# Where TensorE issues the fresh-state products of an attention chunk: behind the other products, or ahead of them

## Time and profile before

| | us |
|---|---|
| median of three runs | 808.82 |
| the three runs | 806.82, 808.82, 809.68 |
| the profiled execution, its own time | 804.45 |
| its span, first to last instruction | 802.5 |
| PE busy in it | 776.2 |
| DVE busy | 536.0 |
| ACT busy | 344.2 |
| POOL busy | 180.3 |

### The profile page before, as it was taken

One profiled execution on the slowest core, in us unless ns is written; L12 is line 12 of the kernel. 1 busy time (PEld: TensorE's weight loads), 2 busy tenths in 40 slices (PEclk: granted clock), 3 DMA queues, 4 the chain that ended last, 5 costly groups with the idle time before them and its releaser, 6 DMA issues.

```text
span 802.5 us, 12138 instructions
## 1 busy us (share of the span) xinstructions
PE 776.2 (97%) x4624; PEld 731.4 (91%) x4624; DVE 536.0 (67%) x1026; ACT 344.2 (43%) x676; POOL 180.3 (22%) x202
## 2 busy tenths in 40 slices
PE   3999999999999999999999999999999999999996
PEld 2769998899999999999999999999999999999996
DVE  7788989865768657666666676676675765553432
ACT  3567554343344343353443443345334444334332
POOL 5515313222213302122212122122221221100000
PEclk9999999999999999999999999999999999999998
DMA  8960222032021221030220311203202030000000
GB/s 227 304 216 1 60 60 60 1 89 60 1 60 30 60 59 31 30 90 1 60 52 9 90 23 37 60 1 89 60 1 60 14 77 30 1 1 29 2 1 33
DMA packets 18849, 43.52 MB, mean 54 GB/s; under 512 B 2272, under 2 KB 14688, under 8 KB 18400
## 3 DMA queue, kind: packets, MB, share of 16 engines
q1 hardware_dynamic: 15136, 34.81, 17.5%
q10 hardware_dynamic: 3648, 7.87, 2.8%
HBM read 37.95 MB, written 4.72 MB: 53 GB/s over the span
## 4 chain that ended last, share of the span: by engine, by line
PE 78%; DVE 2%; ACT 0%; issue 0%; DVEq 0%; ACTq 0%
PE BANKS L1133 55%; PE MISC L1133 20%; PE BANKS L1310 2%; PE MISC L1157 1%; PE MISC L1150 1%; DVE RL L965 0%; DVE Rraw L958 0%; DVE att L818 0%; DVE W2L L976 0%; DVE ki L826 0%; DVE A L839 0%; ACT RH L691 0%; ACT Rraw L687 0%; DVE X2L L982 0%; DVE RL L967 0%
## 5 line engine op out<-in xcount | busy, mean ns | idle before, releaser
L687 ACT ACTIVATE Rraw<-BANKS 128x384 f32<-128x384 f32 x128 | 62.9, 491 | 217.8 <-PE BANKS L1133 217.6
L958 DVE TENSOR_TENSOR Rraw<-BANKS,Rraw 128x384 f32<-128x384 f32 x128 | 71.0, 555 | 118.9 <-ACT Rraw L687 118.8
L1133 PE MATMUL BANKS<-RH,W4H 128*128 128x384 f32 x384 | 135.7, 353 | 0.9 <-DVE RL L965 0.8
L1133 PE MATMUL BANKS<-X2H,W3H 128*128 128x384 f32 x384 | 130.7, 340 | 0.2 <-DVE X2L L982 0.2
L1133 PE MATMUL BANKS<-X2L,W3H 128*128 128x384 f32 x384 | 129.4, 337 | 0.0
L1133 PE MATMUL BANKS<-X2H,W3L 128*128 128x384 f32 x384 | 129.3, 337 | 0.0
L1133 PE MATMUL BANKS<-RH,W4L 128*128 128x384 f32 x384 | 129.2, 337 | 0.0
L1133 PE MATMUL BANKS<-RL,W4H 128*128 128x384 f32 x384 | 129.1, 336 | 0.0
L691 ACT ACTIVATE RH<-Rraw 128x384 fp32r<-128x384 f32 x128 | 67.2, 525 | 94.0 <-DVE Rraw L958 94.0
L965 DVE TENSOR_TENSOR RL<-Rraw,RH 128x384 fp32r<-128x384 f32 x128 | 79.2, 619 | 22.5 <-ACT RH L691 22.5
L826 DVE RECIPROCAL ki<-att 112x128 f32<-112x128 f32 x96 | 89.1, 936 | 0.0
(11 more groups left out here) (137 smaller groups left out, 1486.2 us busy)
## 6 DMA issues: line engine op xcount, KB each, us to landing
att<-rkw SPq DMA_DIRECT2D x48, 288.0 KB, 4.8
out<-OUT SPq DMA_DIRECT2D x8, 576.0 KB, 6.2
rtok<-r_tok SPq DMA_DIRECT2D x22, 192.0 KB, 4.7
ktok<-k_tok SPq DMA_DIRECT2D x22, 192.0 KB, 4.8
vtok<-v_tok SPq DMA_DIRECT2D x22, 192.0 KB, 5.0
W3raw<-w_in ACTq DMA_DIRECT2D x1, 3072.0 KB, 14.6
W4raw<-w_out ACTq DMA_DIRECT2D x1, 3072.0 KB, 18.5
W1raw<-w_in SPq DMA_DIRECT2D x1, 1536.0 KB, 11.5
```

Of the source, the lines that this page charges most:

```text
L687: nc.scalar.activation(Rraw[:, fp % 2, :], PR[fp % 2][:, 0:ST], ACT.Copy, scale=0.01).then_inc(act_slope, 1)
L958: nc.vector.tensor_tensor(Rraw[:, fp % 2, :], PR[fp % 2][:, 0:ST], Rraw[:, fp % 2, :], ALU.max).then_inc(dve_relu, 1)
L1133: return nc.tensor.matmul(dst, lhsT, rhs, start=start, stop=stop, skip_group_check=True)
```

## The change

For the chunks that `item` serves, PE's slot 5 first waits for the tokens and, where the chunk has a fresh state, for the masks of all four pairs; it issues the fresh-state products there, and `attend` behind them. The waits inside `attend` stay, though those for tokens and masks are then already met. Chunks 0 to 2 and the last of each batch keep their order.

```diff
                 if s == 5:
                     wait(pe, act_keT, chunks(b, m, 1, 1))
+                    wait_tok(pe, b, m)
+                    if m % CPB < CPB - 1:
+                        wait(pe, dve_masked, chunks(b, m, PAIRS, PAIRS))
+                        fresh_state(b, m)
                     attend(b, m)
-                    if m % CPB < CPB - 1:
-                        fresh_state(b, m)
```

## The result

The changed kernel takes 814.7 us (median of nine runs, 811.3 to 815.74) against 808.82 for the kernel before on the same chip (nine runs, 804.62 to 810.12). The ratio is 1.0076, 95% interval 1.006 to 1.0091: 6.1 us slower, 4.9 to 7.4. Sign, place and range held; some 1.7 us were not in the sum, and 6.1 lies above the sum's own upper bound of 4.9.

A forecast was written before the change was run, and what follows sets the result against it. TensorE, busy 776.2 of 802.5 us, was taken to bound the kernel. Stalls of 2.45 + 0.97 + 0.55 + 0.41 = 4.4 us on 808.82 gave 813.2, range 809.8 to 815.4.

The forecast's parts named there:

- order of the products, 17 blocks: Same products and weights in another order in slot 5: zero cost, bounded at 0.3 us either way.
- nine blocks with 0.35 or more in hand: Chunks 7, 8, 10, 13, 14, 16, 19, 20, 22: masks end early enough before the first load, so zero cost.
- chunks 9, 12, 15, 18, 21: First chunk of each superstep: first load moves from 0.37 before the masks' end to 0.12 behind, 0.49 each, 2.45 us.
- chunk 4: Masks end 0.92 us after the first load; with 0.12 release 1.04, less 0.07 for the second load: 0.97.
- chunk 6, the wait: TensorE, already idle 1.66 us, waits for the second mask too: first load 0.60 later, taken as 0.55 us.
- chunk 3, the late sum: VectorE gets Y later, so the state starts 0.45 later and TensorE's first expert load moves 0.41 us.
- The release takes 0.12, not 0.05: Time from a mask's end to the load it releases: 0.12 us from chunk 6, 0.05 from chunk 1 as low bound.
- Chunk 6 gives little back at 160.39: TensorE's 0.28 us wait for VectorE's RL could take back up to 0.28 of chunk 6's delay; most comes back.
- A load given back for each wait: Loads pulled ahead past a waiting load would return 0.11 us at each of seven waits, sum 3.6; not adopted.
- Rival 1, taken back: Later TensorE waits (XL, 160.39, behind chunk 9 and its like) absorb 3.2 us, leaving 1.2: 810.0; chance 0.13.
- Rival 2, not felt: Loads run far ahead or release is free; only chunks 3, 4, 6 show parts, under 1.5 us: 810; chance 0.05.
- Rival 3, VectorE's lead: Chunk 4's stall lets VectorE get ahead for good, later waits vanish: -0.7 us, 808.1; chance 0.04.

The follow-up runs named there:

- e3_in_hand: Kernel before with the changed order only in the nine chunks whose masks are 0.35 us or more in hand; 809.31 us against 808.86, ratio 1.0011.
- e2: Changed kernel with the added waits kept at the head of slot 5, but the fresh-state products back behind the A products; 815.02 us, ratio 1.0068 to kernel before.
- e5: Kernel before with one more wait: in chunk 6 slot 5 starts behind both masks; 809.75 us, ratio 1.0012.
- e10: Changed kernel with 18 small useless products on TensorE in front of chunk 6's waits; 812.92 us, ratio 1.0049 to the kernel before.
- e4: Kernel before with the changed order only in chunks 9, 12, 15, 18 and 21; 811.62 us, ratio 1.003.
- e1: Changed kernel, but chunk 6 alone keeps the old order; 813.15 us, ratio 1.0047 to the kernel before.
- e11: Kernel before with the wide products of `cons` ahead of slot 5 in chunks 9, 12, 15, 18 and 21 alone; 805.68 us, ratio 0.9945.
- e7: Changed kernel with `cons` ahead of slot 5 in chunks 4, 6, 9, 12, 15, 18 and 21; 805.46 us, ratio 0.9955 to the kernel before.
- e8: Kernel before with `cons` ahead of slot 5 in chunks 4, 6, 9, 12, 15, 18 and 21; 805.54 us, ratio 0.9956.
- e9: Changed kernel with the wide products of `cons` ahead of slot 5 in chunk 6 alone; 812.27 us, ratio 1.0038 to the kernel before.

## Why the prediction was right, and where its sum was short

Like products, changed kernel against e3_in_hand, how far TensorE falls back at each place:

| step of the prediction | forecast, us | measured, us |
|---|---|---|
| order of the products, 17 blocks | 0 (0.3 either way) | 0 in the nine of e3_in_hand; the others not by themselves |
| nine blocks with 0.35 or more in hand | 0 | 0 (e3_in_hand) |
| chunks 9, 12, 15, 18, 21 | 2.45 | 5 x 0.46 = 2.3 |
| chunk 4 | 0.97 | 1.05 |
| chunk 6, the wait | 0.55 | 0.56 |
| chunk 3, the late sum | 0.41 | 0.36 |
| sum of the waits | 4.4 | 4.3 |
| clock behind chunk 6 | not in the sum | about 2.6 in the profiled execution |

- *The wait is the cost, the move is free.* Right but for chunk 3; e2 and e3 show it one by one.
- *The release takes 0.12, not 0.05.* Right within a hundredth, in chunks 6 and 9 alike; the bound from chunk 1, where loads were still running, was the wrong one of the two. The sentence of the Trainium skill (Perfetto Trace Analysis, Identifying Dependency Chains) stood on the right side: the trace agrees in all seven places, 0.11 or 0.12. No run varies the number of waits alone, though, and it can't be all that counts: with more met waits in between, the load comes 0.07 behind the masks in e5 and 0.18 in e2.
- *Chunk 4, 0.97.* It measured 1.05; the 0.07 taken off for the slot's second load didn't come.
- *Chunk 6 gives little back at 160.39.* Right: in e10, where the clock stayed up, TensorE falls back by 0.6 there, and 0.5 is left from 165 on. The late XL and RL waits moved with TensorE, as argued from ScalarE's 3.57 us of waiting.
- *A load given back for each wait.* Rightly left out of the sum: behind the release in chunk 9 the eight loads of keT take 0.86 us, 0.10 from one to the next, as without a wait before them.
- *Rival 1, taken back.* Refuted by e4. *Rival 2, not felt.* Refuted by the same run. *Rival 3, VectorE's lead.* Its deciding point, 0.49 gained by chunk 9, doesn't come: the lack at chunk 9 is the same as before.
- **The step that failed** is the one for chunk 6: "TensorE already stands idle here, 1.66 us", to which I added 0.6 as time alone. I had read that clock line and this idle stretch, and didn't ask what a longer one does to the clock. It went to the lower level behind it. The runs say 6.1 (4.9 to 7.4) against 4.0 with the idle time filled, so it costs some 2 us in a usual execution, and that covers the difference between 4.4 and 6.1. That the time still fell in the range is luck: the range's upper end allowed for scatter, not for this term. The clock's part isn't the same in each execution: the waits and the clock's part read from the traces of e1 (3.7 and 1.4) and e5 (0.5 and 1.2) make more than their runs measured, 3.8 and 1.0. The short spans of e3_in_hand would account for some 1 us of that, and the mean granted clock of e5's eleven runs lies anywhere from 0.995 to 0.999.

What stays open: where exactly an idle stretch must lie for the clock to fall. e1 and e4_short have the same one (1.39), 1.2 us apart, and only e1's is followed by a fall; no run moves that stretch by itself. Not explained either is a slow drift in the last 50 us of the changed kernel's trace, 0.9 us against e3_in_hand: wide products follow each other at a mean of 0.1767 us instead of 0.1733, with the clock granted at 1.00 in both. The traces of e1, e2, e4 and e10 show it too, and so does e11, which has the old order everywhere; before, e5, e7, e8 and e9 don't. So it isn't the change.

## What to carry to other kernels

When a wait is moved ahead of work that needn't wait, price it from the timeline by how much the releaser lacks at the new place, block by block: here 9 of 17 blocks cost nothing and one kind cost 0.46 each. Where the busiest engine already stands idle once, ask of any change that lengthens it what it does to the clock. And where a short item stands before ready work that another engine waits for, issue the ready work first: five such swaps took 3 to 4 us off, where the order inside the item could only cost.

## What was not expected of the hardware

- Eighteen useless products made the kernel some 2 us faster than without them, since TensorE's granted clock behind them stayed at 1.00 instead of 0.57 over 8 us.
- The clock fell behind 1.39 us of idle TensorE in one kernel (e1_six_old) and not behind the same 1.39 in another (e4_short), where it ended 1.2 us earlier in the span.
- TensorE's first stretch at the lower clock differs in length from one execution to another: the same six products took 2.84 us in one and 5.28 in the other, and what follows it lies 4 us apart, with no change in the code.
